# Fused attention and mixing kernel: TensorE turns y before it turns the probabilities in each attention visit

## The reference, cut to what matters

```python
scores = scale * np.matmul(q, k.transpose(0, 1, 3, 2))
keep = is_sink | in_window                    # 4 sinks, window of 128
scores = np.where(keep, scores, -1000000000.0)
scores = scores - np.max(scores, axis=-1, keepdims=True)
a = np.exp(scores)
a = a / (np.sum(a, axis=-1, keepdims=True) + 1e-09)
attn = np.matmul(a, v)
x = attn.transpose(0, 2, 1, 3).reshape(B, S, H * D)
theta = x @ w_theta
y = w_tok_r over tokens (x * cos(theta)) + w_tok_i over tokens (x * sin(theta))
u = x + y
u = u + np.maximum(u @ w_ch, 0.0)
gate = sigmoid(causal convolution of u, 5 taps)
out = (gate * (u @ w_val)) @ w_out
```

## Time and profile before

| what | value |
|---|---|
| time, median of 3 runs | 663.4 us (662.34 to 663.86) |
| the profiled execution's own time | 665.1 us |
| its span, first to last instruction | 663.3 us |
| PE busy | 643.6 us, 97% |
| DVE busy | 419.3 us, 63% |
| ACT busy | 294.7 us, 44% |
| POOL busy | 253.4 us, 38% |
| attention's steady stretch | about 30 us to 167 us of the span |

### The profile page before, as it was taken

How to read it: one execution, slowest core, us unless ns; L and a number is a source line. 1 busy time by engine, 2 the same in 40 slices (tenths; PEclk the granted TensorE clock), 3 DMA queues, 4 the chain that set the end, 5 groups by cost and what they waited for, 6 DMA issues and landing times.

```text
span 663.3 us, 14158 instructions
## 1 busy us (share of the span) xinstructions
PE 643.6 (97%) x4016; PEld 549.8 (83%) x4016; DVE 419.3 (63%) x1008; ACT 294.7 (44%) x775; POOL 253.4 (38%) x323
## 2 busy tenths in 40 slices
PE   6899999999889999999999999999999999999995
PEld 4677777777778888888888888889999999999994
DVE  4588788778775446463564547778768458458450
ACT  4777777777542322422232323443243243243231
POOL 4455465565142211313131221346355345345320
PEclk9799999999999999999999999999999999999999
DMA  7376666764512135222432237330520220220011
GB/s 247 132 225 203 240 215 208 243 210 164 176 48 65 33 95 161 60 63 79 133 104 60 82 94 240 103 122 1 190 96 30 67 95 28 69 95 26 23 48 52
DMA packets 61048, 76.70 MB, mean 116 GB/s; under 512 B 4176, under 2 KB 41040, under 8 KB 61008
## 3 DMA queue, kind: packets, MB, share of 16 engines
q1 hardware_dynamic: 61008, 76.24, 35.6%
HBM read 51.06 MB, written 25.17 MB: 115 GB/s over the span
## 4 chain that ended last, share of the span: by engine, by line
PE 92%; issue 2%; POOL 2%; DMA 1%; SPq 1%; DVE 1%; ACT 0%; POOLq 0%; DVEq 0%; ACTq 0%
PE acc L1485 30%; PE ps_p L1534 18%; PE ps_o L1574 10%; PE ps_th L1474 10%; PE ps_s L491 7%; PE ps_t L517 7%; PE ps_y L540 7%; PE ps_o L554 2%; PE ps_x L1463 1%; DMA v_sink<-vS 1%; DMA x_res<-xT_scratch 1%; PE ps_o L556 1%; POOL g_lo L1136 0%; POOL z_lo L1104 0%; SPq L1716 0%
## 5 line engine op out<-in xcount | busy, mean ns | idle before, releaser
L1104 POOL TENSOR_TENSOR z_lo<-z_raw,z_hi 128x512 fp32r<-128x512 f32 x48 | 62.5, 1323 | 206.4 <-ACT z_hi L1181 206.4
L1485 PE MATMUL acc<-w2h,z_hi 128*128 128x512 f32 (+1 forms) x384 | 131.2, 342 | 0.9 <-POOL z_lo L1104 0.9
L1485 PE MATMUL acc<-w2l,z_hi 128*128 128x512 f32 (+1 forms) x384 | 129.3, 337 | 0.0
L1485 PE MATMUL acc<-w2h,z_lo 128*128 128x512 f32 (+1 forms) x384 | 129.3, 337 | 0.0
L326 ACT ACTIVATE probs<-masked,neg_max 128x260 f32<-128x260 f32 (+1 forms) x192 | 92.5, 483 | 37.9 <-DVE neg_max L393 25.5
L393 DVE CUSTOM_DVE_ANT_0 masked<-ps_s,mask 128x260 f32<-128x260 f32 (+1 forms) x192 | 69.0, 403 | 39.1 <-PE ps_s L491 32.5
L1485 PEld LDWEIGHTS acc<-w2h,z_hi 128*128 128x128 f32 x384 | 72.8, 190 | 9.0 <-issue 1.2
L1485 PEld LDWEIGHTS acc<-w2h,z_lo 128*128 128x128 f32 x384 | 72.8, 190 | 8.0
L1485 PEld LDWEIGHTS acc<-w2l,z_hi 128*128 128x128 f32 x384 | 72.9, 190 | 7.8
L1295 DVE TENSOR_TENSOR xT_lo<-ps_x,xT_hi 128x512 fp32r<-128x512 f32 x24 | 16.6, 690 | 78.2 <-ACT xT_hi L1165 78.2
L1398 DVE SCALAR_TENSOR_TENSOR ps_g<-m_raw,conv_w,ps_g 128x384 f32<-128x384 f32 x112 | 62.0, 617 | 0.2
(11 more groups left out here) (93 smaller groups left out, 1435.8 us busy)
## 6 DMA issues: line engine op xcount, KB each, us to landing
k_sb<-kT SPq DMA_DIRECT2D x16, 396.0 KB, 3.9
q_sb<-qT SPq DMA_DIRECT2D x16, 384.0 KB, 3.2
v_sb<-vP SPq DMA_DIRECT2D x16, 384.0 KB, 4.5
x_scratch<-x_sb SPq DMA_DIRECT2D x16, 384.0 KB, 2.6
x_nat<-x_scratch SPq DMA_DIRECT2D x24, 256.0 KB, 3.0
xT_scratch<-xT_raw SPq DMA_DIRECT2D x24, 256.0 KB, 2.2
x_res<-xT_scratch SPq DMA_DIRECT2D x24, 256.0 KB, 3.2
uT_scratch<-u_sb SPq DMA_DIRECT2D x24, 256.0 KB, 2.6
```

The lines of the kernel that those rows point to most:

```text
L1104: nc.gpsimd.tensor_tensor(z_lo[s % ZR][:, part, :], z_raw[:, part, :], z_hi[s % ZR][:, part, :].bitcast(F32), ALU.subtract).then_inc(z_lo_ ...
L1485: last = nc.tensor.matmul(bank, l, r, start=first and s == 0 and m == 0 and a == 0, stop=s == T - 1 and m == 1 and a == 2, skip_group_chec ...
```

## The change

In `step` of TensorE the two conditional calls of `turn_y` move ahead of the two of `turn`, in all visits and in the first two pairs as well as in the loop. Nothing else is edited: no wait, no buffer, no other engine's list, and the end behind the loop stays as it was.

```diff
                         if started:
                             pv(n - 1, 1 - s, v, it + s)
+                        if v == 0 and not first:
+                            turn_y(n - 2, s, VISITS - 1)
+                        if v > 0 and started:
+                            turn_y(n - 1, 1 - s, v - 1)
                         if v > 0:
                             turn(n, v - 1, sinks=v == 1 and started)
                         elif started:
                             turn(n - 1, VISITS - 1, False)
-                        if v == 0 and not first:
-                            turn_y(n - 2, s, VISITS - 1)
-                        if v > 0 and started:
-                            turn_y(n - 1, 1 - s, v - 1)
```

## The result

The changed kernel takes 685.13 us (median of 4 runs, 683.49 to 686.36) against 663.05 us before: ratio 1.0332, 95% interval 1.0308 to 1.0356, slower by 22.1 us. The forecast was 686.7 us. Its profiled execution took 684.4 us with a span of 682.5 us.

What follows compares the result with a forecast made beforehand. TensorE's list was taken as the bound. Visit 1 11.9, visit 2 9.8, later VectorE work 2.1 and the start -0.5 sum to 23.3 us; 663.4 + 23.3 = 686.7 us, range 678 to 695.

Steps and rivals of the forecast that it cites:

- Visit 1: Pairs 2 to 15: TensorE stands 0.97 us for normalising, less 0.08 to 0.22 already lost; 14 x 0.85 = 11.9 us.
- Visit 2: Pairs 2 to 15: new wait for normalising, 14 x 0.70 = 9.8 us, plus 2.1 us for later VectorE work.
- The late L414: VectorE's 1e-9 addition, moved later, delays visit 2's first mask by 0 to 0.53 us: 2.1 us in all (0 to 7.4).
- Visit 0: Its turn of y has no wait on normalising, so it swaps places with the turns at no cost.
- The start: Second pair, visit 1: the turn of y fills part of TensorE's 2.09 us wait for ACT, -0.5 us (0 to -0.57).
- The cover: Transposes ahead of the turn of y hide its wait: eight take 1.02 us, visit 1's seven 0.89 of 0.97.
- What the profile was to show: Some 28 L554 waits, 24 to 26 us in all; pair about 11.8 us; clock 1.00; VectorE's wait for scores grows.
- the clock: Rival: new TensorE gaps lower the granted clock in one visit of each of 14 pairs, 704.8 us; chance 0.07.
- The rival of L414: VectorE's addition is caught behind the long POOL instruction in most pairs: 10 lose 0.8 us each, 692.6 us; chance 0.10.
- Only visit 1 paying: Rival: visit 2 hides its wait, so only visit 1's is paid, 674.8 us; chance 0.05.
- The start as decider: Rival: turning y in the start's wait keeps the clock up, giving back 2.7 us; 660.7 at no waits; chance 0.02.

Runs made afterwards that it cites:

- e6: Kernel before, with only VectorE's normalise moved ahead of the four masks of its visit: 659.41 us, ratio 0.9942.
- e2: Kernel before, with the turn of y ahead of the probabilities' turns in the loop's visit 2 alone: 673.55 us, ratio 1.0144.
- e7: Changed kernel without L414, the addition of 1e-9, so that the reciprocal reads the sums directly: 683.22 us, ratio 1.0300.
- e3: Kernel before, with the turn of y ahead of the probabilities' turns in visit 0 alone: 663.32 us, ratio 1.0001.
- e4: Kernel before, with the turn of y first only in the first two pairs, written out before the loop: 663.11 us, ratio 1.0003.
- e8: Changed kernel, but with the turn of y between the two halves of the probabilities' turns: 672.64 us, ratio 1.0138.
- e11: Changed kernel, with normalise moved ahead of the third mask instead of behind the fourth: 665.68 us, ratio 1.0037.
- e5: Changed kernel, with VectorE's normalise moved ahead of the four masks of its visit: 659.99 us, ratio 0.9950.
- e1: Kernel before, with the turn of y ahead of the probabilities' turns in the loop's visit 1 alone: 675.15 us, ratio 1.0171.
- e9: Kernel before, with normalise ahead of the masks and without the addition of 1e-9 (L414): 659.19 us, ratio 0.9943.
- e10: Changed kernel, with normalise ahead of the masks and without the addition of 1e-9 (L414): 659.86 us, ratio 0.9948.

## Why the prediction was right

The direction, the mechanism and the size held: +23.3 us forecast, +22.1 measured. Part of the closeness is luck: visit 1 was put 1.2 us too high, visit 2 0.5 and visit 0 0.3, while the start was counted on for 0.5 us that did not come.

- **Visit 1, forecast +11.9, measured +10.7** (4.20 - 3.44 us, 14 times). The gross wait was right: with no wait at all the visit is 3.23 us, so that the changed kernel loses 4.20 - 3.23 = 0.97 us, the number of the prediction. What I subtracted for the loss that was already there was too small: 0.12 us, between the 0.08 of the chain and the 0.22 of the loads' row, where e6 shows 0.21. The 0.08 came from a pace of 0.128 us for each transpose, which counts the modelled end of the last one; from start to start it is 0.11, and the seven, the first of them somewhat longer, cover 0.82 us in place of 0.89, and the turn of y takes 0.06 us more behind a wait. This is the term that was mis-sized, by 0.09 us a pair.
- **Visit 2, forecast 9.8 + 2.1, measured +11.4.** The wait alone is 4.21 - 3.51 = 0.70 us (e2), as worked out from the lag of 0.05 us. The late L414 is nearly all of the rest: 4.33 - 4.22 = 0.11 us (the full change against e7), 1.5 us in 14 visits against 2.1 forecast. The spread and its cause are shown by e2, which has no spread with visit 1 untouched, and e7, which has none without L414.
- **Visit 0, forecast 0, measured -0.3 in the loop**, and nothing in e3's time. It is two small things: 0.03 us more by the order (e3), and the alternation with 3.16 us gone, as also in e2, where the order of visit 0 is the old one.
- **The start, forecast -0.5, measured about 0.** e4's time, 0.2 us more than the kernel before with an interval of about 1 us to each side, does not resolve it, but the traces at full clock do. The turn of y now stands in the wait, and visit 2 of the second pair begins at 20.14 us (20.50 in e3, which has the old order there and got ScalarE's probabilities 0.14 us later). But that visit then takes 4.21 us where e3's takes 3.83, and the third pair begins at 24.35 against 24.33. The prediction saw no new wait in that visit, since it had only the half clock's rows to count from; at full clock the loads of L554 wait for L426 there too, 0.31 us, and the values wait 0.49 us for ScalarE's copy of y (0.28 in e3).
- **The cover.** e8 and e11 change only how much stands ahead of the wait on TensorE, or ahead of normalise on VectorE. The cost follows both, and vanishes in e5. The rival that the order in itself costs is out as the cause of the 22 us; what is left of it is some 0.05 us a pair. e8 came out 1.1 us above its forecast, by the same pace of 0.128 us in place of 0.11.
- **What the profile was to show.** The clock of 1.00, the 28 waits and a pair of 11.6 us (11.8 forecast) are there. The loads' waits are 1.13 and 0.87 us in the pair shown and 29.8 us in all, where I had forecast 0.9 to 1.0, 0.7 to 0.85 and 24 to 26: I worked out lost time, and the row has the 0.17 us beside it that e5 shows. One sign was wrong: VectorE's wait for scores did not grow but fell from 23.3 to 12.1 us (28 to 170 us), and what it waits for instead are the transposes, 21.0 us, which it never waited for before.

The rivals: the clock stayed at 1.00 in the steady stretch, so that the frequent waits of 0.7 to 1.0 us between groups of matmuls did not bring it down. The Trainium skill ("TensorE: Matmul & The Clock Gate", section "A second HAM failure mode: psum-queue depth-cycling") tells of a kernel whose clock swung with frequent short idles between such groups; this trace does not show it. The rival of L414 had its condition right and its price wrong: it was caught behind an L294 in 10 of 14 pairs, but mostly near that instruction's end, so that only two visits 2 lost about 0.5 us, and all of it is 1.5 us and not 8. Only visit 1 paying is refuted by e2. The start as decider is refuted by e4.

## What to carry to other kernels

A wait that is "nearly covered" in the profile is the place at which to count before an order is touched: take its releaser's end, subtract the moment at which the new order would arrive there and what the old order already loses, and that is the loss per pass. Count the cover from start to start of the instructions, not to a modelled end: here 0.11 us and not 0.128 for each transpose. Then look at the releaser's own list before the waiter's: here the work waited for stood behind four instructions that did not need it, in an engine that was idle just ahead of them, and moving it up was worth more (25.1 us on the changed kernel, 4.1 us on the old one) than any order on the waiting engine. A single small wait row of 0.22 us, 14 times, was worth reading as real time (0.21), although the busy rows showed a full engine. Such a row is still no measure by itself: in the changed kernel the loads' rows of 1.13 and 0.87 us stood for 0.97 and 0.70 us lost, and only a version without the wait told how much to take off.

## What the runs showed of the hardware

- An add over 12 numbers a lane took 160 to 903 ns, by what GpSimd was doing when it started (L414 in the kernels before, after and e1), and up to 1231 ns in e5. Whenever it was long, it ended about 0.03 us behind a cast or a tensor_tensor of GpSimd that had started before it. Where the GpSimd instruction started after it, it took its 0.16 us (134.03 us of the kernel before, with a cast from 134.09).
- Right behind products with the values, a weight load read 0.17 us idle with nothing to wait for (e5), and two transposes took 0.37 us behind a wait against 0.31 without one (before and e6).
- After the start's wait of TensorE for ACT the granted clock went to 0.50 for some microseconds in some executions and stayed at 1.00 in others, with the same order (e1 and e3). It fell in the six profiles where that wait read 1.42 to 2.61 us (before, e1, e2, e5, e6, e8) and stayed in the seven where it read at most 1.04 (after, e3, e4, e7, e9, e10, e11). It is worth up to 2.6 us of a profiled span, so a profile's span should not be compared with another's below that without looking at the clock by stretch.
- In the changed kernel's steady stretch TensorE was idle for about 15% of the time (102.42 us busy of 120), in pieces of 0.6 to 1.2 us by the rows of its matmuls, and the clock was 1.00 throughout.
